# Later places in the queues for dependent operations of the first block and the attention, and other places for the token loads of layer 2

## The reference, cut to what matters

```python
q_s = exp(q - max(q, -1)); q_s = q_s / (sum(q_s, -1) + 1e-9)
k_s = exp(k - max(k, 2));  k_s = k_s / (sum(k_s, 2) + 1e-9)
kv = einsum('bhsd,bhse->bhde', k_s, v)
x = einsum('bhsd,bhde->bhse', q_s, kv)        # -> 4608 x 512
g = x @ w_gate                                # 512 x 1536
y = (g * sigmoid(g) * (x @ w_val)) @ w_out    # layer 1
h = max(max(y @ w1, y @ w2), y @ w3)          # layer 2, 512 x 768
out = h @ w_out2
```

## Time and profile before

| | |
|---|---|
| Median of 3 runs | 1571.32 us (1570.8 to 1578.69) |
| Profiled execution | 1575.45 us, of it 1573.7 us span |
| PE busy | 1501.4 us, 95% of the span |
| DVE, POOL, ACT busy | 817.0, 655.3, 543.5 us |
| Granted TensorE clock, mean | 0.982 |
| First block, gate 0 to product 0.7 | 37.9 to 230.1 us |
| Pairs 0 to 2, with attention | to 828.7 us |
| Layer 2 starts | 1008.2 us |

### The profile page before, as it was taken

How to read it: one execution, slowest core, us unless ns; L and a number is a source line. 1 busy time by engine, 2 the same in 40 slices (tenths; PEclk the granted TensorE clock), 3 DMA queues, 4 the chain that set the end, 5 groups by cost and what they waited for, 6 DMA issues and landing times.

```text
span 1573.7 us, 20750 instructions
## 1 busy us (share of the span) xinstructions
PE 1501.4 (95%) x7002; PEld 1241.0 (79%) x7002; DVE 817.0 (52%) x1344; ACT 543.5 (35%) x996; POOL 655.3 (42%) x523
## 2 busy tenths in 40 slices
PE   8787779999999999999999999999989999999999
PEld 7665667787777888888888888888778888888898
DVE  6545446575576654755455444634533443453444
ACT  5434234353443433443233222533421322322322
POOL 5547356564743324433143132787831241231221
PEclk9989899999999999999999999999999999999999
DMA  8968448577585765655556644287494575565585
GB/s 239 329 218 281 150 171 266 205 245 253 201 273 183 224 224 193 199 182 189 179 190 197 227 154 148 84 318 261 187 351 130 168 265 166 177 229 174 173 304 200
DMA packets 180903, 334.56 MB, mean 213 GB/s; under 512 B 13376, under 2 KB 68672, under 8 KB 173120
## 3 DMA queue, kind: packets, MB, share of 16 engines
q1 hardware_dynamic: 175616, 323.80, 62.4%
q10 hardware_dynamic: 5184, 9.44, 1.9%
HBM read 256.90 MB, written 76.28 MB: 212 GB/s over the span
## 4 chain that ended last, share of the span: by engine, by line
PE 80%; POOL 7%; DVE 4%; issue 3%; ACT 3%; DMA 1%; SPq 1%; ACTq 0%; DVEq 0%; POOLq 0%
PE round L1561 12%; PE round L1564 11%; PE round L1563 11%; PE y_bank L1589 8%; PE y_bank L1590 8%; PE y_bank L1591 8%; PE third_bank L1561 5%; PE third_bank L1564 5%; PE third_bank L1563 5%; PE att_bank L1494 2%; POOL wring L586 1%; POOL h L606 1%; PE att_bank L1499 1%; POOL q_sb L555 1%; PE att_bank L1506 1%
## 5 line engine op out<-in xcount | busy, mean ns | idle before, releaser
L606 POOL TENSOR_TENSOR h<-hid,h 128x512 fp32r<-128x512 f32 (+1 forms) x156 | 202.6, 1302 | 444.0 <-ACT h L1083 443.7
L1561 PE MATMUL round<-xops,wring 128*128 128x512 f32 (+1 forms) x930 | 358.1, 385 | 10.3 <-ACT round L1028 6.8
L1564 PE MATMUL round<-xops,wring 128*128 128x512 f32 (+1 forms) x930 | 353.5, 380 | 0.0
L1563 PE MATMUL round<-xops,wring 128*128 128x512 f32 (+1 forms) x930 | 353.4, 380 | 0.0
L1364 DVE TENSOR_TENSOR y_sb<-y_sb,y_bank 128x512 f32<-128x512 f32 x232 | 158.3, 684 | 227.5 <-PE y_bank L1591 227.0
L1561 PEld LDWEIGHTS round<-xops,wring 128*128 128x128 f32 x930 | 175.5, 189 | 47.2 <-ACT round L1028 8.6
L1564 PEld LDWEIGHTS round<-xops,wring 128*128 128x128 f32 x930 | 175.3, 189 | 33.7
L1563 PEld LDWEIGHTS round<-xops,wring 128*128 128x128 f32 x930 | 175.7, 189 | 31.6
L1083 ACT ACTIVATE h<-hid 128x512 fp32r<-128x512 f32 (+1 forms) x156 | 95.4, 612 | 193.6 <-DVE hid L1325 116.6
L1589 PE MATMUL y_bank<-h,wout 128*128 128x512 f32 x384 | 152.2, 396 | 0.0
L1591 PE MATMUL y_bank<-h,wout 128*128 128x512 f32 x384 | 150.3, 391 | 0.0
(11 more groups left out here) (161 smaller groups left out, 2608.2 us busy)
## 6 DMA issues: line engine op xcount, KB each, us to landing
wring<-kept SPq DMA_DIRECT2D x216, 512.0 KB, 4.1
wout<-kept_o SPq DMA_DIRECT2D x36, 1024.0 KB, 6.8
wring<-kept SPq DMA_DIRECT2D x108, 256.0 KB, 3.4
stage<-x_dram SPq DMA_DIRECT2D x32, 512.0 KB, 5.8
kept<-wring SPq DMA_DIRECT2D x9, 1792.0 KB, 8.5
kept<-wring SPq DMA_DIRECT2D x12, 1024.0 KB, 6.1
raw<-w_g SPq DMA_DIRECT2D x21, 512.0 KB, 4.7
x_dram<-stage SPq DMA_DIRECT2D x16, 576.0 KB, 3.6
```

The lines of the kernel that those rows point to most:

```text
L606: pool.tensor_tensor(h[:, t, 1, 0:cols], hid[:, t, 0:cols], h[:, t, 0, 0:cols].bitcast(F32), ALU.subtract).then_inc(h_lo_ready, 1)
L1561: pe.matmul(dst[:, 0:g.cols], hi, x1, start=(i in (1, 5) and c == 0), stop=False, skip_group_check=True)
L1563: pe.matmul(dst[:, 0:g.cols], hi, x2, start=False, stop=False, skip_group_check=True)
L1564: mm = pe.matmul(dst[:, 0:g.cols], lo, x1, start=False, stop=(c == 1), skip_group_check=True)
```

## The change

It moves instructions inside the queues, and changes no instruction. In the first block ACT's tanh and DVE's two steps move from `at_once` to `next_after`, the split of h on ACT to two events after `val`, its low part on DVE to three. So they stand behind the weight splits (ACT) and behind `max_k`, `max_q`, `sum_q` (DVE) of the next event. POOL's weight splits, `subtract_q` and `scale_q` move one event later, `split_kv` three. ACT reads out KM and KV two events after the item, DVE reads out QT two after.

The places of a batch change: QT3 to QT5 move one place earlier, X0 to X3 and X5 to X7 by half a place or less, and X4 stands 2.6 places behind QT5 (before: one). `exp_q` stands 1.6 and `sum_q` 3.2 places behind `max_q` (before: 0.8 and 2.0). The two batches of the first block get 28 instead of 31 units of its length, and the loads and splits of pair 0 move with them. In layer 2 the loads for pair 5 move three groups earlier (from group 53 to 50), and for pairs 6 to 8 two groups later (for pair 6 from group 57, the first of its pair, to 59), with their `sum_x` two groups later (59 to 61); for pair 5 `sum_x` stays.

```diff
-GAPS = [4, 7, 8, 9, 10, 11, 13, 14, 15, 16, 17, 18, 19, 20, 21, 23, 24, 25, 26, 27, 28, 29]
-TASKS = {0: [("K", 0), ("Q", 0)], 1: [("K", 1)], 2: [("K", 2), ("Q", 1)], 3: [("K", 3), ("Q", 2)],
-         4: [("Q", 3)], 5: [("Q", 4)], 6: [("Q", 5)]}
+GAPS = [4, 7, 8, 9, 10, 11, 13, 14, 15, 16, 17, 18.5, 19.3, 20.1, 20.9, 22, 23, 24, 26.6, 27.5, 28.4, 29.3]
+MAX_K = [2.5, 5.5, 8.5, 11.5]
+MAX_Q = [2.6, 8.6, 11.6, 14.6, 17, 19.2]
...
-                events.append((3 * j + 2.6, ("max_q", b, n)))
-                events.append((3 * j + 3.4, ("exp_q", b, n)))
-                events.append((3 * j + 4.6, ("sum_q", b, n)))
+        events += [(place, ("max_q", b, n)), (place + 1.6, ("exp_q", b, n)), (place + 3.2, ("sum_q", b, n))]
...
-              (3 * 10 + 1.2, ("load_x", 0, 1)), (3 * 11 - 0.2, ("sum_x", 0))]
-    timed += [(3 * 11 + 0.2 + k, ("split_x", 0, o)) for k, o in enumerate((1, 3))]
+              (28.3, ("load_x", 0, 1)), (29.2, ("sum_x", 0))]
...
-    timed = spread(timed, (1, 2), 31)
+    timed = spread(timed, (1, 2), 28)
...
-            timed += [(1.5 + k, ("split_x", 0, o)) for k, o in enumerate((4, 5, 6))]
+            timed += [(0.6 + k, ("split_x", 0, o)) for k, o in enumerate((1, 3, 4, 5, 6))]
...
-            early = 0 if pair < 3 or pair == PAIRS1 else 5
+            early = 0 if pair < 3 else 3
...
-            timed.append((where["product", final - 1 - early, 1] + 0.3, ("sum_x", pair + 1)))
+            timed.append((where["product", final - 1 - (0 if pair == PAIRS1 else early), 1] + 0.3,
+                          ("sum_x", pair + 1)))
...
@@ block.gpsimd, next_after and third_after
+                if e[0] == "gate" and e[1] + 2 < F1:
+                    split_unit(3 * (e[1] + 2))
...
                 elif e[0] == "max_q":
                     subtract_q(e[1], e[2])
                 elif e[0] == "sum_q":
                     scale_q(e[1], e[2])
...
+            def third_after(e):
+                if e[0] == "item" and ITEMS[e[2]][0] == "KV":
+                    split_kv(e[1], ITEMS[e[2]][1])
...
@@ block.scalar
             def at_once(e):
                 if e[0] == "gate":
-                    first_tanh(e[1])
                     if e[1] + 2 < F1:
                         split_unit(3 * (e[1] + 2))
                 elif e[0] == "val":
-                    first_split_h(e[1])
...
             def next_after(e):
-                if e[0] == "item":
+                if e[0] == "gate":
+                    first_tanh(e[1])
+                elif e[0] == "item" and ITEMS[e[2]][0] == "QT":
                     item_out(e[1], e[2])
...
+            def second_after(e):
+                if e[0] == "val":
+                    first_split_h(e[1])
+                elif e[0] == "item" and ITEMS[e[2]][0] in ("KM", "KV"):
+                    item_out(e[1], e[2])
...
@@ block.vector
             def next_after(e):
-                if e[0] == "item":
+                if e[0] == "gate":
+                    first_gate(e[1])
+                elif e[0] == "val":
+                    first_value(e[1])
+                elif e[0] == "item" and ITEMS[e[2]][0] != "QT":
                     item_out(e[1], e[2])
...
             def second_after(e):
-                if e[0] == "product":
+                if e[0] == "item" and ITEMS[e[2]][0] == "QT":
+                    item_out(e[1], e[2])
...
+            def third_after(e):
+                if e[0] == "val":
+                    first_h_low(e[1])
```

More of the change, by code:

```diff
@@ L194, in batch_places @@
         events.append((place, ("item", b, n)))
[L195 to L199, removed]
-                events.append((3 * j + 2.6, ("max_q", b, n)))
-                events.append((3 * j + 3.4, ("exp_q", b, n)))
-                events.append((3 * j + 4.6, ("sum_q", b, n)))
+    events += [(place, ("max_k", b, n)) for n, place in enumerate(MAX_K)]
+    for n, place in enumerate(MAX_Q):
+        events += [(place, ("max_q", b, n)), (place + 1.6, ("exp_q", b, n)), (place + 3.2, ("sum_q", b, n))]
     return events
@@ L627, in at_once @@
             def at_once(e):
[L628 to L633, removed]
+                if e[0] == "first_weights":
                     if e[1]:
@@ L645, in at_once, with next_after @@
                         combine_weights(n + 2)
+            def next_after(e):
+                if e[0] == "gate" and e[1] + 2 < F1:
+                    split_unit(3 * (e[1] + 2))
+                elif e[0] == "val" and e[1] + 2 < F1:
+                    split_unit(3 * (e[1] + 2) + 1)
+                    split_unit(3 * (e[1] + 2) + 2)
                 elif e[0] == "max_q":
@@ L649, in at_once @@
                     scale_q(e[1], e[2])
-            def next_after(e):
-                if e[0] == "item" and ITEMS[e[2]][0] == "KV":
-                    split_kv(e[1], ITEMS[e[2]][1])
                 elif e[0] == "split_x" and e[2] % 2 == 1:
@@ L674, in _ @@
                 next_after(earlier(n - 1))
+                third_after(earlier(n - 3))
             next_after(order[-1])
@@ L1190, in _ @@
                 next_after(earlier(n - 1))
+                second_after(earlier(n - 2))
             next_after(order[-1])
@@ L1265, in first_value, with first_h_low @@
                    .then_inc(hidden_ready, 1)
+            def first_h_low(j):
                 dve.wait_ge(first_h_hi, j + 1)
@@ L1372, in at_once @@
             def at_once(e):
[L1373 to L1377, removed]
+                if e[0] == "second" and e[1] == F1 - 1:
                     first_results()
@@ L1408, in second_after @@
             def second_after(e):
-                if e[0] == "product":
+                if e[0] == "item" and ITEMS[e[2]][0] == "QT":
+                    item_out(e[1], e[2])
+                elif e[0] == "product":
                     _, n, i = e
```

## The result

The changed kernel takes 1558.44 us (median of 7 runs, 1552.79 to 1563.07), against 1571.42 for the kernel before (7 runs). The ratio is 0.9904, with a 95% interval of 0.9883 to 0.9925: faster by 1%, where 1543 was forecast and 1558 lies in the range of 1524 to 1562. The profiled execution took 1555.91 us with a span of 1554.1, so 19.5 us less than the profiled one of before; the medians are 13 apart.

What follows compares the result with a forecast made beforehand. PE was busy 95% of the span; order, not work, made it wait or run at half speed. Gains 8 + 9.3 + 5 + 7.4 = 29.7 us from 1575.45 gave 1545.7, taken as 1543 us for the runs; range 1524 to 1562.

Steps and rivals of the forecast that it cites:

- The signs that were named: Waits and start times expected in the profile after, at KM0, QT2, X4, product 0.2, product 0.7, SP's queue and the `y`.
- Layer 2: Token loads and `sum_x` placed later remove PE's 5.48 us wait for h at 1180.60: 7.4 us, bounds 0 to 7.5.
- The end of the block: First block's end: earlier load and sums for pair 0 remove nearly all idle and clock loss: 9.3 us, bounds 5 to 11.
- The block: First block's attention: 3.7 us less idle and 4.2 us of clock, together 8 us, bounds -6 to 50.
- Attention in the pairs: Pairs 0 to 2: X4 waits go, some QT2 and QT5 waits come; net 5 us, bounds -8 to 9.
- The slower rival: `scale_q` behind POOL's waits for h holds PE at two QT items in seven batches: 38 us lost, 1579 us, chance 0.04.
- the first rival: New waits (port, ACT, late `scale_q` at QT2 and QT5) eat the attention's gain, block and pairs 0: 1555 us, chance 0.2.
- The term against it: First block: DVE's small additions lose the shared SBUF port to POOL, 8 us on DVE, 3 us of it on PE's way.

Runs made afterwards that it cites:

- l2_only: The kernel before with only the change's layer 2 (and pair 4) places of `load_x` and `sum_x`: 1565.99 us, ratio 0.9959.
- no_l2: The changed kernel with `load_x` and `sum_x` of pairs 4 to 8 placed as before: 1564.21 us, ratio 0.9943.
- tail_only: The kernel before with only the first block's two batches in 28 units and pair 0's loads, sums and splits placed as in the change: 1578.34 us, ratio 1.0031.
- places_only: The changed kernel's order of events, layer 2 as before, with every engine's `at_once` and `next_after` as before: 1584.33 us, ratio 1.0071.
- scale_at_once: The changed kernel with `scale_q` on POOL back in `at_once`, one event earlier: 1545.75 us, ratio 0.9823.
- pairs_sum_early: The changed kernel with `exp_q` and `sum_q` 0.8 and 2.0 places behind `max_q`, as before, for batches 3 to 7: 1537.31 us, ratio 0.9785.
- q2_early: The changed kernel with `max_q`, `exp_q` and `sum_q` of QT2 1.2 and of QT5 1.0 places earlier, all batches: 1536.51 us, ratio 0.9771.

## Why the prediction was right or wrong

**In direction and range right, in size too high**: 13 us by the medians for 28 forecast, 19.5 for 29.7 by the profiled executions. By the traces 10.2 us are missing: 12.7 in the pairs with attention, less some 2.4 that the other parts gave above their terms. The signs that were named came, among them KM0 at 3.5 us, QT2 released by `q_sb`, X4 gone from the waits of the pairs, and no wait at product 0.2 or at the `y`.

- **Layer 2**: right in mechanism and size, 8.2 us for 7.4. Shown by l2_only and no_l2, for the loads and `sum_x` together.
- **The end of the block**: 9.0 us for 9.3 from product 0.1 to 0.7. Right as a stretch. As a term of its own it was wrong: tail_only gains 7 there and loses as much in front in its trace, more by the medians.
- **The block**: 9.9 us for 8. Its waits are 30.0 us where 29.6 were counted, the half-speed stretches 23.9 us, 12 lost, for a forecast of 12.7. Single places were off by more than the sum: KM0 3.54 (3.7 forecast), X4 1.98 (2.4), KV1 of batch 2 1.94 (3.1), KM3 of batch 2 4.03 (3.3), QT2 6.71 and 2.85 (2.8 and 4.8). The errors cancelled, and the sum is better than its parts. That it agrees so well is in part luck, since traces of one block differ by up to 2.7 us. One reading of the working was wrong as well: of DVE, ACT and POOL, all were to be busy under half of the block's windows, but POOL is busy for 54% of the second and 67% of the third, and after the change for all of the window at the block's end.
- **Attention in the pairs: the step that failed.** "QT2 of batch 3 0.6, others 1 together. Net 9.0 - 4.1". The 6.35 us at X4 went as said, and QT5 of batch 3 was right to 0.3 us. But QT2 waits 2.38 us in batch 3 and 1.8 to 2.9 in three more, QT5 2.8 in batch 4 too: 14.9 us for 4.1. All waits of this part grew by 6.0 us, and the half-speed stretches doubled, from 6.8 to 13.7 us (3.4 lost, for 1.7 gained in the forecast). That is -7.7 us for +5, at the lower bound that was given (-8). The slower rival named this very mechanism and gave it 0.04: it came at 15 us in place of 38. So did the first rival (0.2, 1555 us), with QT2 and QT5 in its list; it was right on the pairs and on the time, and wrong on the block, which it put at 0. With -7.7 in place of +5 the forecast would have been near 1556. To find that, two chains had to be followed in every batch: the scaling behind POOL's split of h (QT5 of batch 3), and the sum behind a read-out on DVE that waits for ACT (QT5 of batch 4).
- **The term against it**, POOL working closer behind DVE, was given 3 us and left out of the sum. For the additions that it was worked out from it did not come. Their mean from 40 to 216 us fell from 453 ns to 326:

```profile
L1219 DVE TENSOR_SCALAR q_sum_eps<-q_sum 96x8 f32<-96x8 f32 x13 | 4.2, 326 | 0.4
```

  Whether other operations of the two engines met more often was not looked at.
- What the prediction did not separate, the runs do: the places cost 11 us by themselves (places_only), and the queue moves on ACT and DVE turn that into a gain; POOL's moves bring the block nothing, and its later scaling costs 13 (scale_at_once).

## What to carry to other kernels

An instruction that waits for a long chain belongs behind those that are ready (here on ACT: 9 us in the block for the tanh, the split of h and two kinds of read-out; DVE's share was not measured). But each place later also shortens the distance to the consumer: after such a move, write down for every consumer, in every repetition of the pattern, how many products lie between and what stands ahead of each step in its queue, and move the producers of the short ones up (21 us here, more than the whole change). An order that is denser in one place frees time in another only if the chains in it have slack; try the two apart.

## What the runs showed of the hardware

A 96x8 addition on DVE took 0.17 us with POOL idle (at 265.04 in the changed kernel) and 1.12 us while POOL subtracted. The load of one unit of weights took 4.0 us at 41 us in the kernel before and 6.3 us at 67 us in the changed one, with the DMA engines busy 0.86 of the time from 42 to 113 us in either kernel; one number for all places in a kernel is not to be had from one row.

Half-speed stretches of PE came right behind waits of 2.2 to 2.9 us, or began in them: in the pairs of the changed kernel there are four of 3.4 us each, at QT2 of batches 3, 5 and 6 and at QT5 of batch 4. Not each such wait has one: QT5 of batch 3 waited 2.80 us and the clock stayed at its upper level. Where the waits went (scale_at_once, pairs_sum_early, q2_early) the stretches went as well, and this is why pairs_sum_early gained 21 us where its waits in the pairs are only 13 less.
